# Attention on transposed 64x64 tiles, its root spread by DMA, in a fused attention and two-expert kernel

## The chip, the cores and the metric

One Trainium2 chip, one core of it. The metric is the device time of one launch in microseconds, the median of three runs.

## What is computed

Linear attention over 8 batches, 8 heads, 576 rows, 64 columns a head, an RMS norm over each head's 64 columns, a gated layer with a product over the rows, then a convolution layer, all in fp32.

```python
kv = einsum('bhsd,bhse->bhde', k, v)
o = einsum('bhsd,bhde->bhse', q, kv)
x = o / sqrt(mean(o * o, -1) + 1e-6) * g_norm          # heads joined: (8, 576, 512)
h = relu(x @ w_in); u, v = halves of h
v_n = (v - mean(v)) / sqrt(var(v) + 1e-6)
x = (u * (w_spatial @ v_n + b_spatial)) @ w_out        # first layer
h = relu(x @ w_in2)
c = convolution of h over the rows, 3 taps
out = (h * sigmoid(c)) @ w_out2                        # second layer
```

## The kernel before, in words

The program is written by hand, one instruction list for each engine, tied by semaphores: what stands in a list runs in that order, and a wait holds everything behind it on its engine. `PE` is TensorE, `DVE` VectorE, `ACT` ScalarE, `POOL` GpSimd, and `SP` the queue that issues the loads and stores.

The products of the two layers are made of three products each (`PASSES`): both factors are split into a high part (a copy rounded to fp32r, `HI`) and a low part (the rest, `LO`). The attention's own products are plain fp32. Each plain fp32 matmul leaves two MATMUL and two LDWEIGHTS records in the trace, a transpose or an fp32r matmul one of each.

The program has three stages. **The prologue** (to 44.4 us) loads and splits the weights, multiplies `w_out` by `w_in2` (`W`, L435 and `w_product`, 96 matmuls of 512 columns) and begins the attention of batch 0. **The first stage** (to about 457 us) is `body(b)` for the eight batches: the value product `v_product(b, i)` in five tiles of rows (L358), the product `u_product(b, m)` in four tiles of columns and the product over the rows `spatial_product(b, m)` in four (both L337), with the attention of batch b+1 laid between them. **The second stage**, to the end, is the second layer; it has no attention.

In the attention of a batch, `kv_product` makes k^T v for a pair of heads at a time on the whole 128x128 array (L312, 20 matmuls of 128 columns); `kv_copy` (L796) takes the two diagonal blocks out. `o_product(a, i)` multiplies 128 rows of q by it (L323, 4 matmuls; five times a batch), rows on the partitions. ACT copies and squares the result (L541, L543), DVE sums each head's squares (L802), forms the mean, takes the root's inverse with one Newton step (L812 to L820), ACT has made the root (L548), and DVE scales the rows (L823). `x_transpose(a, i)` (L330, 4 a time) turns them, since the layer's product wants columns on the partitions; ACT makes the high part (L558) and DVE the low part (L833) with the factor g. In `body` of TensorE, `attend(b + 1)` hands out one of these pieces ahead of `u_product(b, 2)` and one ahead of each `spatial_product`, the last transpose in the next body. SP loads k and v of batch b+2 and q once the products that read them are done, and stores each gated tile (`store_gated`, into a scratch in DRAM).

A bank group written by one product waits for its readers: `spatial_product(b, 3)` for `gate(b, 0)`, the value product for `gate` of the batch before.

## Time and profile before

| | |
|---|---|
| median of three runs | 862.21 us (861.88 to 862.80) |
| the profiled execution, its own time | 862.53 us |
| its span, first to last instruction | 860.3 us |
| TensorE busy | 840.8 us, 98% |
| VectorE, ScalarE, GpSimd busy | 501.5, 394.3, 42.1 us |
| chain that ended last | TensorE 96% |
| granted TensorE clock, mean | 0.994 |

Busy time of TensorE is modelled: each record is longer than the distance to the next one's start, since matmuls overlap in the pipeline. What a matmul costs a full TensorE is read from the starts. The time between the span and the execution's own time, 2.2 us, is launch and end.

### The profile page before, as it was taken

How to read it: one execution, taken by the hardware profiler on the slowest of the kernel's cores; microseconds unless marked ns; L12 is line 12 of the kernel's file. 1: busy time of each engine (PE TensorE's matmuls, PEld its weight loads, DVE VectorE, ACT ScalarE, POOL GpSimd, SP SyncE). 2: the span in 40 equal slices, each digit the busy share in tenths (PEclk: the TensorE clock that was granted, in tenths of full speed). 3: DMA queues.
4: the chain of work that ended last, by engine and by line, in shares of the span. 5: the costliest groups of instructions: out<-in, count | busy, mean ns of one | idle time of the engine just before them, and what ended most of it. 6: DMA issues, size and time to landing. Idle time of an engine off the chain costs nothing.

```text
span 860.3 us, 14580 instructions
## 1 busy us (share of the span) xinstructions
PE 840.8 (98%) x5408; PEld 781.4 (91%) x5408; DVE 501.5 (58%) x1184; ACT 394.3 (46%) x718; POOL 42.1 (5%) x42
## 2 busy tenths in 40 slices
PE   6969999999999999999999999999999999999998
PEld 5859989899998999999899899898989989898996
DVE  3577775756767576675746828174561828347380
ACT  5435343342434434344354637274552738356461
POOL 4151000000000000000022000000000000000000
PEclk9979999999999999999999999999999999999999
DMA  9812322233302323221202030120203020120101
GB/s 312 276 56 85 97 76 93 93 110 110 109 28 82 123 96 110 81 84 70 83 26 86 1 105 2 54 63 37 69 13 104 0 100 4 40 76 3 46 0 61
DMA packets 26276, 65.88 MB, mean 77 GB/s; under 512 B 2050, under 2 KB 2050, under 8 KB 24196
## 3 DMA queue, kind: packets, MB, share of 16 engines
q1 hardware_dynamic: 26100, 65.45, 22.2%
q8 instruction: 19, 0.31, 0.1%
q14 instruction: 13, 0.11, 0.0%
q10 hardware_dynamic: 144, 0.01, 0.0%
HBM read 46.58 MB, written 18.87 MB: 76 GB/s over the span
## 4 chain that ended last, share of the span: by engine, by line
PE 96%; DVE 1%; POOL 1%; ACT 1%; DMA 0%; issue 0%; SPq 0%; POOLq 0%; ACTq 0%; DVEq 0%
PE ps L337 49%; PE ps L492 23%; PE ps L358 11%; PE ps L312 4%; PE ps L323 4%; PE ps L330 2%; PE ps L435 2%; PE ps L447 1%; POOL w_in_split L285 1%; DMA sq_xn<-w_in_dram 0%; POOL w_in_split L276 0%; POOL w_in_split L280 0%; DVE sq_xn L823 0%; DVE ssq L802 0%; DVE rm L816 0%
## 5 line engine op out<-in xcount | busy, mean ns | idle before, releaser
L337 PEld LDWEIGHTS ps<-x_gated_split,w_product_split 128*128 128x128 f32 x1536 | 204.3, 188 | 0.5
L337 PE MATMUL ps<-x_gated_split,w_product_split 128*128 128x288 f32 x1536 | 204.8, 295 | 0.0
L492 PE MATMUL ps<-w_in_split,v_hg_split 128*128 128x512 f32 x832 | 194.6, 390 | 0.0
L492 PEld LDWEIGHTS ps<-w_in_split,v_hg_split 128*128 128x128 f32 x832 | 155.8, 188 | 31.9
L961 DVE SCALAR_TENSOR_TENSOR work<-work,const_cols 128x576 f32<-128x576 f32 x64 | 52.4, 819 | 150.0 <-ACT work L733 149.9
L337 PE MATMUL ps<-w_sp_split,v_hg_split 128*128 128x288 f32 x896 | 126.0, 298 | 0.0
L337 PEld LDWEIGHTS ps<-w_sp_split,v_hg_split 128*128 128x128 f32 x896 | 120.0, 188 | 0.0
L337 PE MATMUL ps<-x_gated_split,w_in_split 128*128 128x288 f32 x768 | 105.5, 297 | 0.0
L337 PEld LDWEIGHTS ps<-x_gated_split,w_in_split 128*128 128x128 f32 x768 | 102.5, 188 | 0.2
L358 PE MATMUL ps<-w_in_split,x_gated_split 128*128 128x512 f32 x384 | 94.3, 402 | 2.0 <-POOL w_in_split L276 2.0
L358 PEld LDWEIGHTS ps<-w_in_split,x_gated_split 128*128 128x128 f32 x384 | 73.1, 194 | 17.2 <-POOL w_in_split L276 2.2
L728 ACT ACTIVATE work<-ps 128x576 f32<-128x576 f32 x64 | 41.8, 653 | 70.6 <-PE ps L337 57.2
L802 DVE TENSOR_REDUCE ssq<-sq_xn 128x8 f32<-128x512 f32 (+1 forms) x40 | 27.4, 684 | 74.8 <-ACT sq_xn L543 74.7
L764 ACT ACTIVATE sq_xn<-ps 128x512 f32<-128x512 f32 x32 | 19.1, 598 | 85.0 <-PE ps L492 85.0
L541 ACT ACTIVATE sq_xn<-ps 128x512 f32<-128x512 f32 (+1 forms) x40 | 23.8, 595 | 64.2 <-PE ps L323 64.2
L967 DVE SCALAR_TENSOR_TENSOR work<-work,const_cols 128x576 f32<-128x576 f32 x64 | 52.1, 815 | 0.6
L733 ACT ACTIVATE work<-work,const_cols 128x576 f32<-128x576 f32 x64 | 49.9, 779 | 2.1
L972 DVE TENSOR_TENSOR work<-work 128x576 f32<-128x576 f32 x64 | 48.2, 753 | 0.1
L567 ACT ACTIVATE work<-ps 128x512 f32<-128x512 f32 x32 | 19.1, 598 | 57.8 <-PE ps L358 46.5
L843 DVE BATCH_NORM_STATS2 bn_stats<-work 128x6 f32<-128x512 f32 (+1 forms) x40 | 27.6, 689 | 28.1 <-ACT work L567 22.5
L978 DVE TENSOR_TENSOR v_hg_split<-work,v_hg_split 128x512 fp32r<-128x512 f32 x64 | 43.9, 685 | 0.0
L738 ACT ACTIVATE work<-work 128x576 f32<-128x576 f32 x64 | 42.9, 670 | 0.0
(90 smaller groups left out, 847.3 us busy)
## 6 DMA issues: line engine op xcount, KB each, us to landing
kv_raw<-kv_main_dram SPq DMA_DIRECT2D x8, 2048.0 KB, 8.7
q_raw<-q_T_dram SPq DMA_DIRECT2D x8, 1152.0 KB, 5.9
gated_scratch<-work SPq DMA_DIRECT2D x32, 288.0 KB, 2.1
q_raw<-gated_scratch SPq DMA_DIRECT2D x8, 1152.0 KB, 5.5
out_dram<-sq_xn SPq DMA_DIRECT2D x32, 256.0 KB, 2.0
work<-w_in_dram SPq DMA_DIRECT2D x3, 1024.0 KB, 8.2
kv_raw<-kv_rest_dram SPq DMA_DIRECT2D x8, 256.0 KB, 9.0
kv_raw<-w_out_dram SPq DMA_DIRECT2D x1, 2048.0 KB, 8.1
```

Source lines behind the costliest of these rows:

```text
L312: last = pe.matmul(PS[:, OB, n], KV[:, 0, j, n], KV[:, 1, j, n], start=(j == 0), stop=(j == NT - 1))
L323: last = pe.matmul(PS[:, OB, m * P:(m + 1) * P], QP[:, o:o + P], kvbd[:, m, :], start=True, stop=True)
L337: last = pe.matmul(pair[bank][:, c, :], st, mo[:, c * HALF:(c + 1) * HALF], start=(n == 0), stop=(n == len(steps) - 1))
L358: last = pe.matmul(dst, x, w, start=(n == 0), stop=(n == len(st) - 1))
L492: last = pe.matmul(PS[:, ROW_BANK[i], :], x, wout2[:, w, f, :], start=(f == 0 and n == 0), stop=(f == FT - 1 and n == len(PASSES) - 1))
L728: act.activation(whole(h_sb[f % 3][:, 1:S + 1]), pair[f % 3], ACT.Relu).then_inc(s_hr, 1)
L733: act.activation(t_sb[f % 2], h_sb[f % 3][:, 1:S + 1], ACT.Copy, scale=cols[:, FT + f:FT + f + 1]).then_inc(s_t0, 1)
L738: act.activation(p_sb[f % 2], t_sb[f % 2], ACT.Sigmoid).then_inc(s_sig, 1)
L961: dve.scalar_tensor_tensor(out=t, in0=h[:, 0:S], scalar=cols[:, f:f + 1], in1=t, op0=ALU.mult, op1=ALU.add).then_inc(s_cv1, 1)
L967: dve.scalar_tensor_tensor(out=t, in0=h[:, 2:S + 2], scalar=cols[:, 2 * FT + f:2 * FT + f + 1], in1=t, op0=ALU.mult, op1=ALU.add).then_inc ...
L972: dve.tensor_tensor(p_sb[f % 2], h_sb[f % 3][:, 1:S + 1], p_sb[f % 2], ALU.mult).then_inc(s_mul, 1)
L978: dve.tensor_tensor(hg[LO][:, f, :], p_sb[f % 2][:, 0:w], hg[HI][:, f, :].bitcast(F32), ALU.subtract).then_inc(s_hlo, 1)
```

## The change

All of the attention is rewritten so that it gives o transposed, with the head's columns on the partitions:

- `kv_product` makes one head at a time, 64x64, the two heads of a pair in the left and right half of the array's columns (40 matmuls of 64 columns a batch, same bank, other partitions). ACT and DVE copy the blocks, each twice (to partitions 0 to 63 and 64 to 127).
- `o_product(a, m)` makes o^T for a pair of heads: four matmuls of 64x64 weights and 288 columns, for two halves of the rows (on the array's two halves of rows) and two heads (on its two halves of columns). 16 a batch. They write banks 6 and 7, which ACT copies to `o_T` (`o_copy`) before the next m.
- ACT squares `o_T` (`square`). `square_sum(a, m)` sums the squares over the partitions by a matmul with a matrix of ones in one column (`sel`): eight matmuls of 64 rows by 32 columns of weights and 144 moving columns, each in another eighth of the array, 32 a batch, into banks 4 and 5.
- There are no transposes. The inverse root is made once a batch on 128x288 elements, written to a scratch in DRAM by four DMAs, and read back by two DMAs that give each of the 64 partitions of a head the same row (`spread_r`). DVE then scales `o_T` by it and by g (`x_scale`, four of 576 elements); ACT makes the high part (`x_hi`), POOL the low part (`x_lo`) and the left-over rows (`x_rows_left`).
- On TensorE `kv_product(b + 1)` stands at the body's start, and `o_product` and `square_sum` between the value products. Their waits are put on the last matmul of the value product ahead of them. Body 0 has an order of its own (`first_body`); the batches 1 to 6 are the loop, batch 7 has no attention to make.
- On SP k, v and q of batch 0 are loaded ahead of the last halves of the weights, and the root of batch 0 is waited for between weight loads.
- Eleven plain fp32 matmuls on zeros start as soon as DVE has filled them, before the weights are there (`s_warm`).
- The buffers of the old path are gone or laid over others; banks change (`V_BANK`).

The core of the diff:

```diff
+V_BANK = [0, 1, 2, 3, 2]
 ROW_BANK = [6, 7, 4, 6, 7]
+KV_BANK, SSQ_BANK, O_BANK = 5, 4, 6
...
+        sq = sb("o_squared", [P, 2, S])
+        rB = sb("r_spread", [P, MT, S])
+        sel = sb("head_select", [P, MT, 32])
+        ms, std, r0 = (sb(n, [P, CH, QS]) for n in ("ms", "std", "r0"))
...
+            def spread_r(a):
+                sp.wait_ge(s_r, a + 1)
+                for g in range(4):
+                    sp.dma_start(r_dram[a, :, :, g * QS:(g + 1) * QS].rearrange("c m t -> m c t"),
+                                 r0[g * 32:g * 32 + MT, :, :]).then_inc(s_rst, DMA)
+                sp.wait_ge(s_rst, (a + 1) * 4 * DMA)
+                for c in range(CH):
+                    rows = r_dram[a, c].rearrange("m s -> (m s)").partition_broadcast(D)
+                    sp.dma_start(rB[c * D:(c + 1) * D, :, :].rearrange("p m s -> p (m s)"), rows).then_inc(s_rB, DMA)
...
+            load_w0(0)
+            load_w0(1)
             load_kv(0)
             load_q(0)
+            load_w0(2)
+            load_w0(3)
+            sp.dma_start(w2_raw[1], w2[:, :, F1:F2]).then_inc(s_w21_in, DMA)
+            sp.wait_ge(s_woT, MT)
+            sp.dma_start(wv_raw, w[:, :, F1:F2]).then_inc(s_win_in, DMA)
+            spread_r(0)
...
             with sp.Fori(0, B - 2) as b:
                 sp.wait_ge(s_kv, b + 2)
                 load_kv(b + 2)
-                store_gated(b, 0, 2)
-                sp.wait_ge(s_o, (b + 2) * NT)
+                sp.wait_ge(s_o, (b + 2) * MT)
                 load_q(b + 2)
-                store_gated(b, 2, MT)
+                spread_r(b + 1)
+                store_gated(b, 0, MT)
...
+            def x_lo(a, m):
+                pool.wait_ge(s_xhi, a * MT + m + 1)
+                pool.tensor_tensor(XG[:, LO, m, :], o_T[:, m, :], XG[:, HI, m, :].bitcast(F32), ALU.subtract).then_inc(s_x, 1)
+
+            def x_rows_left(a):
+                pool.wait_ge(s_xhi, (a + 1) * MT)
+                left = slice(FULL * P, S)
+                pool.tensor_tensor(x_rest[:, :, REST:P], o_T[:, :, left], XG[:, HI, :, left].bitcast(F32), ALU.subtract)
+                pool.tensor_copy(x_rest[:, :, 0:REST], XG[:, HI, :, left].bitcast(F32)).then_inc(s_xr, 1)
...
+            with pool.Fori(2, B) as a:
+                for m in range(MT):
+                    x_lo(a, m)
+                x_rows_left(a)
...
             def kv_product(a):
-
                 pe.wait_ge(s_kv_in, (a + 1) * KV_LOADS * DMA)
-                pe.wait_ge(s_sq, a * NT)
-                for hp in range(MT):
-                    n = slice(hp * P, (hp + 1) * P)
+                for m in range(MT):
                     for j in range(NT):
-                        last = pe.matmul(PS[:, OB, n], KV[:, 0, j, n], KV[:, 1, j, n], start=(j == 0), stop=(j == NT - 1))
+                        for c in range(CH):
+                            n = slice((m * CH + c) * D, (m * CH + c + 1) * D)
+                            last = pe.matmul(PS[c * D:(c + 1) * D, KV_BANK, m * D:(m + 1) * D], KV[:, 0, j, n], KV[:, 1, j, n],
+                                             start=(j == 0), stop=(j == NT - 1))
                 last.then_inc(s_kv, 1)
 
-            def o_product(a, i):
-                if i == 0:
+            def o_ready(a, m):
+                if m == 0:
                     pe.wait_ge(s_q_in, (a + 1) * DMA)
-                    pe.wait_ge(s_kvbd, a + 1)
-                else:
-                    pe.wait_ge(s_sq, a * NT + i)
-                for m in range(MT):
-                    o = m * S + i * P
-                    last = pe.matmul(PS[:, OB, m * P:(m + 1) * P], QP[:, o:o + P], kvbd[:, m, :], start=True, stop=True)
+                    pe.wait_ge(s_kvd0, a + 1)
+                    pe.wait_ge(s_kvd1, a + 1)
+                pe.wait_ge(s_oc, a * MT + m)
+
+            def o_product(a, m):
+                if isinstance(a, int):
+                    o_ready(a, m)
+                for half in (0, 1):
+                    r = slice(half * D, (half + 1) * D)
+                    for c in range(CH):
+                        last = pe.matmul(PS[c * D:(c + 1) * D, O_BANK + half, 0:HALF], kvd[r, m, c, :], QR[r, m, c, :],
+                                         start=True, stop=True)
                 last.then_inc(s_o, 1)
 
-            def x_transpose(a, i):
-                pe.wait_ge(s_norm, a * NT + i + 1)
-                pe.wait_ge(s_x, a * NT + i)
-                for m in range(MT):
-                    last = pe.transpose(PS[:, TB, m * P:(m + 1) * P], xn[i % 2][:, m * P:(m + 1) * P], ident[:, :])
-                last.then_inc(s_xtp, 1)
+            def square_ready(a, m):
+                pe.wait_ge(s_sq, a * MT + m + 1)
+
+            def square_sum(a, m):
+                if isinstance(a, int):
+                    square_ready(a, m)
+                for g in range(4):
+                    for c in range(CH):
+                        r = slice(c * D, (c + 1) * D)
+                        last = pe.matmul(PS[g * 32:(g + 1) * 32, SSQ_BANK + c, 0:QS], sel[r, m, :], sq[r, m % 2, g * QS:(g + 1) * QS],
+                                         start=(m == 0), stop=(m == MT - 1))
+                last.then_inc(s_ssq, 1)
...
                 for n, (x, w) in enumerate(st):
+                    if n == len(st) - 1 and ahead and not isinstance(b, int):
+                        if i < MT:
+                            o_ready(b + 1, i)
+                        if i:
+                            square_ready(b + 1, i - 1)
...
             def body(b, ahead):
-                first = isinstance(b, int) and b == 0
+                if ahead:
+                    pe.wait_ge(s_g, b * MT - 2)
+                    kv_product(b + 1)
                 for i in range(NT):
-                    if i == 2:
-                        x_transpose(b, 4)
-                    v_product(b, i)
-                    if first and i == 0:
-                        o_product(0, 4)
-                        x_transpose(0, 3)
-                if ahead and not first:
-                    kv_product(b + 1)
-                if first:
-                    pe.wait_ge(s_winu, MT)
-                u_product(b, 0)
-                u_product(b, 1)
-                pieces = attend(b + 1) if ahead else iter(())
-                if first:
-                    kv_product(1)
-                    u_product(b, 2)
-                    next(pieces)
-                else:
-                    next(pieces, None)
-                    u_product(b, 2)
-                u_product(b, 3)
-                if first:
-                    pe.wait_ge(s_sp_lo, NT)
-                    pe.wait_ge(s_b, 1)
+                    v_product(b, i, ahead)
+                    if ahead:
+                        if i < MT:
+                            o_product(b + 1, i)
+                        if i:
+                            square_sum(b + 1, i - 1)
                 for m in range(MT):
-                    next(pieces, None)
+                    u_product(b, m, ahead)
+                for m in range(MT):
                     spatial_product(b, m)
...
+            pe.wait_ge(s_warm, 1)
+            for n in range(11):
+                pe.matmul(PS[:, O_BANK, 0:P], sq[:, 0, 0:P], sq[:, 0, 0:P], start=True, stop=True)
+            for j in (0, 1):
...
+            def o_copy(a, m):
+                act.wait_ge(s_o, a * MT + m + 1)
+                if not (isinstance(a, int) and a == 0):
+                    act.wait_ge(s_x, a * MT)
+                    act.wait_ge(s_xr, a)
+                act.activation(whole(o_T[:, m, :]), PS[:, O_BANK:O_BANK + 2, 0:HALF], ACT.Copy).then_inc(s_oc, 1)
+
+            def square(a, m):
+                act.wait_ge(s_oc, a * MT + m + 1)
+                act.wait_ge(s_ssq, a * MT + max(m - 1, 0))
+                act.activation(sq[:, m % 2, :], o_T[:, m, :], ACT.Square).then_inc(s_sq, 1)
+
+            def x_hi(a, m):
+                act.wait_ge(s_xm, a * MT + m + 1)
+                if m == 0:
                     act.wait_ge(s_u, a * MT)
-                src = PS[:, TB, :].rearrange("p (m t) -> p m t", m=MT)[:, :, 0:n]
-                if i == FULL:
-                    act.activation(x_rest[:, :, 0:n], src, ACT.Copy, scale=g_col)
-                act.activation(XG[:, HI, :, i * P:i * P + n], src, ACT.Copy, scale=g_col).then_inc(s_xhi, 1)
+                act.activation(XG[:, HI, m, :], o_T[:, m, :], ACT.Copy).then_inc(s_xhi, 1)
...
+            def square(a, m):
+                dve.wait_ge(s_oc, a * MT + m + 1)
+                dve.wait_ge(s_ssq, a * MT + max(m - 1, 0))
+                dve.tensor_tensor(sq[:, m % 2, :], o_T[:, m, :], o_T[:, m, :], ALU.mult).then_inc(s_sq, 1)
+
+            def mean_square(a):
+                dve.wait_ge(s_ssq, (a + 1) * MT)
+                dve.tensor_scalar(ms[:, :, :], PS[:, SSQ_BANK:SSQ_BANK + CH, 0:QS], 1.0 / D, EPS,
+                                  ALU.mult, ALU.add).then_inc(s_ms, 1)
+
+            def inverse_root(a):
+
+                dve.wait_ge(s_std, a + 1)
+                dve.wait_ge(s_rst, a * 4 * DMA)
+                dve.reciprocal(r0[:, :, :], std[:, :, :]).then_inc(s_nr, 1)
...
+                dve.wait_ge(s_nr, a * 4 + 4)
+                dve.tensor_tensor(r0[:, :, :], r0[:, :, :], std[:, :, :], ALU.mult).then_inc(s_r, 1)
+
+            def x_scale(a, m):
+                if m == 0:
+                    dve.wait_ge(s_rB, (a + 1) * CH * DMA)
+                    dve.wait_ge(s_sq, (a + 1) * MT)
+                dve.scalar_tensor_tensor(out=o_T[:, m, :], in0=o_T[:, m, :], scalar=g_col, in1=rB[:, m, :],
+                                         op0=ALU.mult, op1=ALU.mult).then_inc(s_xm, 1)
...
             def body(b, ahead):
+                if ahead:
+                    kv_copy(b + 1)
                 for i in range(NT):
                     v_stats(b, i)
-                    if isinstance(b, int) and b == 0 and i == 0:
-                        mean_square(0, 4)
-                        x_lo(0, 3)
-                        normalise(0, 4)
                     if i:
                         v_lo(b, i - 1)
-                    if i == 1:
-                        x_lo(b, 4)
                     v_normalise(b, i)
+                if ahead:
+                    mean_square(b + 1)
                 v_lo(b, NT - 1)
-                if isinstance(b, int) and b == 0:
-                    dve.wait_ge(s_b_hi, 1)
-                    dve.tensor_tensor(wspB[96:97, :], b_raw[96:97, :], wspB[96:97, :].bitcast(F32),
-                                      ALU.subtract).then_inc(s_b, 1)
                 if ahead:
-                    kv_copy(b + 1)
-                pieces = attend(b + 1) if ahead else iter(())
-                next(pieces, None)
+                    inverse_root(b + 1)
+                    for m in range(MT):
+                        x_scale(b + 1, m)
                 for m in range(MT):
-                    next(pieces, None)
                     if not ahead and m == 2:
                         gated_lo(0, 0)
                         gated_lo(0, 1)
                     gate(b, m)
```

TensorE, one body of the loop (batches 1 to 6). Before:

```order
L358 MATMUL ps<-w_in_split,x_gated_split 128x512 x12
...
L358 MATMUL ps<-w_in_split,x_gated_split 128x512 x12
...
L330 MATMUL ps<-ident,sq_xn 128x128 x4
...
L358 MATMUL ps<-w_in_split,x_gated_split 128x512 x24
L358 MATMUL ps<-w_in_split,rest_split 128x512 x8
...
L312 MATMUL ps<-kv_raw 128x128 x20
L337 MATMUL ps<-x_gated_split,w_in_split 128x288 x48
...
L323 MATMUL ps<-kv_blocks,q_raw 128x128 x4
L337 MATMUL ps<-x_gated_split,w_in_split 128x288 x24
...
L337 MATMUL ps<-x_gated_split,w_in_split 128x288 x24
...
L323 MATMUL ps<-kv_blocks,q_raw 128x128 x4
L330 MATMUL ps<-ident,sq_xn 128x128 x4
```

Now (L355 is the k^T v product, L372 o^T, L385 the sums of squares, L422 the value product, L393 `u_product` and the product over the rows):

```order
L355 MATMUL ps<-kv_raw 64x64 x40
...
L422 MATMUL ps<-w_in_split,x_gated_split 128x512 x11
...
L422 MATMUL ps<-w_in_split,x_gated_split 128x512
L372 MATMUL ps<-q_raw,kv_double 64x288 x4
L422 MATMUL ps<-w_in_split,x_gated_split 128x512 x11
...
L422 MATMUL ps<-w_in_split,x_gated_split 128x512
L372 MATMUL ps<-q_raw,kv_double 64x288 x4
L385 MATMUL ps<-o_squared,head_select 32x144 x8
L422 MATMUL ps<-w_in_split,x_gated_split 128x512 x11
```

The 20 + 20 + 20 instructions of the attention (two of every three plain fp32) have become 40 + 16 + 32, all plain fp32, in fifteen changes between tiles of the whole array and of parts of it a body, where there was one size.

VectorE, the end of one body of the loop, from the left-over rows' value statistics on. Now:

```order
L890 TENSOR_SCALAR ms<-ps 128x288
L952 TENSOR_TENSOR v_hg_split<-work,v_hg_split 64x512
...
L897 RECIPROCAL r<-std 128x288
...
L899 TENSOR_TENSOR std<-r 128x288
...
L901 TENSOR_TENSOR std<-std,ms 128x288
...
L903 TENSOR_SCALAR std<-std 128x288
...
L905 TENSOR_TENSOR r<-r,std 128x288
...
L911 SCALAR_TENSOR_TENSOR o_x<-o_x,const_cols,r_spread 128x576 x4
...
L957 TENSOR_TENSOR work<-ps,work 128x576
...
L957 TENSOR_TENSOR work<-ps,work 128x576
```

The four scalings by the spread root (L911) stand ahead of the four gates (L957) that the product over the rows and the stores wait for. Before, a gate followed each tile's normalisation (L823), and no DMA was waited for.

The queue of SP, one turn of its loop. Now:

```order
L181 DMA q_raw<-q_T_dram 128x2304
...
L186 DMA r_scratch<-r 4x2x144
...
L186 DMA r_scratch<-r 4x2x144
...
L186 DMA r_scratch<-r 4x2x144
...
L186 DMA r_scratch<-r 4x2x144
...
L191 DMA r_spread<-r_scratch 64x2304
...
L191 DMA r_spread<-r_scratch 64x2304
...
L196 DMA gated_scratch<-work 128x576
```

The root's four writes and two reads stand between the load of q and the stores of the gated tiles.

## Rows read from the trace of the kernel before

**Rows 1.** The page: busy time by engine, and the chain that ended last.

```profile
PE 840.8 (98%) x5408; PEld 781.4 (91%) x5408; DVE 501.5 (58%) x1184; ACT 394.3 (46%) x718; POOL 42.1 (5%) x42
...
PE 96%; DVE 1%; POOL 1%; ACT 1%; DMA 0%; issue 0%; SPq 0%; POOLq 0%; ACTq 0%; DVEq 0%
```

**Rows 2.** Windows, bodies 1 to 6: length, TensorE busy, clock, DMA.

```profile
106.94:158.41 51.47, 51.47 (x367) 1.00 0.27 92
...
364.30:415.77 51.47, 51.47 (x366) 1.00 0.22 80
```

**Rows 3.** Order of time, TensorE, body 1: start us, us, line, count.

```profile
120.15 4.62 PE L312 MATMUL ps<-kv_raw 128*128 128x128 f32 x40
124.53 6.60 PE L337 MATMUL ps<-x_gated_split,w_in_split 128*128 128x288 f32 x48
130.97 1.05 PE L323 MATMUL ps<-kv_blocks,q_raw 128*128 128x128 f32 x8
131.78 6.61 PE L337 MATMUL ps<-x_gated_split,w_in_split 128*128 128x288 f32 x48
138.22 1.05 PE L323 MATMUL ps<-kv_blocks,q_raw 128*128 128x128 f32 x8
139.11 0.60 PE L330 MATMUL ps<-ident,sq_xn 128*128 128x128 f32 x4
139.47 3.96 PE L337 MATMUL ps<-w_sp_split,v_hg_split 128*128 128x288 f32 x28
...
158.41 0.86 PE L358 MATMUL ps<-w_in_split,x_gated_split 128*128 128x512 f32 x3
```

**Rows 4.** Groups by line, TensorE's weight loads: busy us, mean ns.

```profile
L312 PEld LDWEIGHTS ps<-kv_raw 128*128 128x128 f32 x320 | 36.8, 192 | 1.7 <-issue 1.2
L330 PEld LDWEIGHTS ps<-ident,sq_xn 128*128 128x128 f32 x160 | 19.1, 143 | 8.7 <-DVE sq_xn L823 7.7
```

**Rows 5.** Windows, prologue and body 0, TensorE.

```profile
0.00:44.44 44.44, 34.74 (x180) 1.00 0.84 285
44.44:106.94 62.50, 56.79 (x377) 0.92 0.23 78
```

**Rows 6.** Waits of TensorE in the whole span: us, times, longest.

```profile
PE ps L330 <- DVE sq_xn L823: 6.7, 3, 5.7
PE ps L435 <- DVE w_product_split L926: 5.8, 1, 5.8
PE ps L358 <- POOL w_in_split L276: 2.0, 1, 2.0
```

**Rows 7.** Windows: length, TensorE busy, granted clock, DMA share, GB/s.

```profile
5.00:10.00 5.00, 4.17 (x10) 1.00 0.98 324
...
58.00:60.00 2.00, 1.20 (x5) 0.50 0.00 0
...
62.00:64.00 2.00, 2.00 (x10) 0.89 0.00 0
```

**Rows 8.** Groups, first weight product, 5 to 12 us, then 12 to 19.

```profile
L435 PE MATMUL ps<-w_product_split,v_hg_split 128*128 128x512 f32 x16 | 6.4, 583 | 5.8 <-DVE w_product_split L926 5.8
...
L435 PE MATMUL ps<-w_product_split,v_hg_split 128*128 128x512 f32 x33 | 7.7, 390 | 0.0
```

**Rows 9.** Page, DMA issues: count, KB each, median us to landing.

```profile
q_raw<-q_T_dram SPq DMA_DIRECT2D x8, 1152.0 KB, 5.9
gated_scratch<-work SPq DMA_DIRECT2D x32, 288.0 KB, 2.1
```

**Rows 10.** Groups by line, VectorE and GpSimd: busy us, mean ns.

```profile
L961 DVE SCALAR_TENSOR_TENSOR work<-work,const_cols 128x576 f32<-128x576 f32 x64 | 52.4, 819 | 150.0 <-ACT work L733 149.9
L876 DVE TENSOR_TENSOR work<-ps,work 128x576 f32<-128x576 f32 x32 | 24.2, 755 | 12.4 <-PE ps L337 12.3
...
L290 POOL TENSOR_TENSOR w_sp_split<-w_sp_raw,w_sp_split 128x576 fp32r<-128x576 f32 x4 | 5.7, 1419 | 13.8 <-ACT w_sp_split L666 13.8
```

**Rows 11.** Loads of q, issue to landing.

```profile
DMA to landing us min/median/max: 5.2/5.9/16.3
```

458 lines of the change are left out of this document (239 added, 219 removed).

## The prediction

> **What bounds the kernel now.** I read the page first: TensorE is busy 98% of the span and 96% of the chain that ended last, all others at 58% or less [rows 1]. Then the stretches of the first stage: each of bodies 1 to 6 lasts 51.47 us, TensorE is busy in all of it, its clock is granted in full, and the DMA engines are at a quarter [rows 2]. So in the loop only what TensorE executes counts. Then the order of time of one body, for the price of the attention by starts: k^T v 124.53 - 120.15 = 4.38 us for 40 records; the pieces of o, of which a body has five, 0.81 once and then 0.89 each, 4.37 us for 40; the five transposes 0.36 each, 1.8 us for 20 [rows 3]. Together 10.5 us of a body, seven times, and the rest, 41.0 us, is untouched by the change. Last the start, where TensorE does idle: the prologue has 34.7 us of work in 44.4, body 0 lasts 62.5 us, 11.0 more than its sisters, with 56.8 busy [rows 5]. The waits there are 5.8 us for the first weights, 5.7 of the 6.7 before transposes in one wait for VectorE's scaled rows, and 2.0 for GpSimd [rows 6]. Around them the clock is at its lower level: granted 0.50 from 58 to 60 us, 0.89 from 62 to 64 [rows 7]. The second stage is not touched.
>
> **The unit price.** A record of a plain fp32 matmul with 128 columns costs 4.38 / 40 = 0.110 us [rows 3], 0.86 ns a column, and every such matmul leaves two. By columns, then, a record of the new k^T v (64 columns) is 0.055 us, of o^T (288) 0.246, of the sums of squares (144) 0.123. A batch has 80, 32 and 64 of them: 4.4, 7.9 and 7.9 us if they run one after the other. Side by side in the halves, quarters and eighths of the array, they are 2.2, 2.0 and 1.0 us. The trace of before has only tiles of the whole array and shows neither. The bounds of the sum are thus 5.2 and 20.2 us a batch, against 10.5.
>
> **Which value I take.** I take the tiles to run side by side, with three allowances. For k^T v a record is preceded by its weight load, 192 ns for 128 columns, which today just hides under the neighbours at one per 0.110 us [rows 3, 4]; halved it is as long as the halved record, so it may or may not be shared: 3.3 us, the middle of 2.2 and 4.4. For o^T 2.2 us (2.0 and a little for four ends). For the sums of squares a start every 0.015 us would be needed to reach 1.0; the closest starts in the trace are those of the transposes, 0.36 / 4 = 0.09 us [rows 3], which at 64 records would be 5.8 us. I take 2.2, nearer the lower end, since starts at 0.09 are only an upper bound of what issue needs. Then there are fifteen changes of tile size a body. None is in the trace. The lower bound is 0; the upper, from the weight load that can't hide and is followed by its matmul, 0.19 us each [rows 4], 2.9 us in all. I take 0.1 each, 1.5 us. Sum: 3.3 + 2.2 + 2.2 + 1.5 = 9.2 us, 1.3 less than 10.5.
>
> The Trainium skill (TensorEngine Tiling, Key Properties) says that changing the tiling mode drains the array, but gives no time; no run here shows it yet. By it the fifteen changes can't be free.
>
> **The loop.** Six bodies by -1.3: -7.9 us. This holds if nothing new makes TensorE wait. Each cover by name. The copies of k^T v (two of 256 elements on each of two engines, less than the 0.76 us of one with 576 [rows 10]) lie under the first value product, 2.7 us (24 of 512 columns in 5.5). `o_copy` and `square` on ScalarE, priced by the same row at 0.76 us each at most, lie under the next value product, whose last matmul carries the wait; behind that wait stands the whole of TensorE, the margin is about 1 us. The root: the sums end about 21.9 us into the body; mean, root, Newton step and the low part between them are eight instructions of some 0.48 us (288 elements, under two thirds of 0.76 [rows 10]), 3.8 us; the writes 2.1 us and the spread of 1152 KB 5.9 us [rows 9] end it at about 34.5; four scalings of 0.82 [rows 10] end at 37.8. The first gate behind them on VectorE is due when its spatial product is done, at 38.6, and TensorE needs it at 46.2. The low parts, 4 x 1.42 us on GpSimd [rows 10], and the left-over rows end at about 45, and the next value product starts after 53. If that cover of 8 us were gone, the rest would fall on each of seven bodies. On SP the spread stands ahead of the stores, which ScalarE waits for only a body later: nothing. Whatever VectorE and ScalarE are relieved of is worth nothing beside a full TensorE.
>
> **The start.** The first weight product now finds its clock up. Its first 16 records last 583 ns, the later 33 last 390 [rows 8]; 48 matmuls take 13.7 us for 10.9 at the later pace of 0.228. The eleven matmuls on zeros are 22 records at twice 0.110 us, 4.8 us, and end at about 5.7, where the first weights are there. Nothing is behind them. The order of loads: 1.05 MB of weights and 2.36 of k and v at 324 to 428 GB/s [rows 7] are there at about 12.5 us. The prologue's sum: 5.8 of waiting, 96 weight products x 0.228 = 21.9, attention 9.2, a wait of 1.5 for k and v, 4 for copies that nothing covers (`kv_copy`, three times `o_copy` with one pair of banks), ends at 42.4 us. But x of batch 0 needs the seventh piece of W, done 2.7 earlier, then two copies 1.5, four scalings 3.3, the parts 2.1, so the first value product is at 46.6, after an idle of 4 us that lowers the clock again: the window at half clock before cost some 1.7 us each time [rows 7], and I take that. With 1.8 us for waits that I don't see, body 0 begins at 48.4 and takes 41.0 + 9.2 + 1.7, and body 1 begins at 100 instead of 106.9: -6.9. What goes is the stall of 5.7 us for VectorE; what is late next is x.
>
> **Sum.** 862.5 - 7.9 - 6.9 = 847.7 us against the profiled execution (862.53; its span is 860.3, with 2.2 us around it). The median of the runs is 0.3 lower: 847.5, I say 848. Own range of this case 830 to 858.
>
> **Rivals.**
>
> *Two records, one tile: only neighbours overlap.* Each matmul is two records for the same tile, and the second can't start before the first has streamed. If starts keep their order, the next tile's first record can lie only beside this tile's second: each matmul costs one record instead of two, and one at the end. Then o^T is 4 x 5 x 0.246 = 4.9 us, the sums 4 x 9 x 0.123 = 4.4, with 3.3 and 1.5 together 14.1 us a batch, 3.6 more than now. Six bodies: +21.6; the start, with about 1.7 batches of attention 4.9 dearer, -6.9 + 8.3 = +1.4. Time: 885 us, slower. With free changes of tile and k^T v at 2.3 it is 866, so the case decides from two tiles on that can't share. For it: starts are in order in every row of rows 3, and a record's pair is always adjacent. Against it: nothing in the trace but that a part of the array is idle. The Trainium skill (TensorE: Matmul & The Clock Gate, Part 3) states that matmuls keep program order in start and end, and measures side-by-side tiles at 3.07 times for four; it does not say what two passes of fp32 do. By that order the sum would be this rival's.
>
> *No overlap at all.* 20.2 + 1.5 = 21.7 us a batch: six bodies +67, the start -6.9 + 21, so 944 us. For it: only that no row shows tiles side by side.
>
> *The spread is late.* One load of q took 16.3 us to land instead of 5.9 [rows 11]; the spread reads one short row for 64 partitions. At 16.3 us the scalings end at 48.2, the gate that TensorE needs at 46.2 comes at 49, and each of seven bodies stands 3 us: 848 + 21 = 869. Below 13 us it costs nothing.
>
> *The change only moves work*, 10.5 us a batch as before: -6.9 by the start alone, 856.
>
> **How the numbers follow.** Side by side: 0.52. Only neighbours: 0.30. None: 0.08. Late spread: 0.05. Only the start: 0.05. The time is that of the first, 848. The range goes down to 828, a little under its own range (side by side with free changes and cheap k^T v is 5.2 us a batch, 817, and leaves 0.06 out), and up to 890, which holds the neighbours' 885 and leaves out its upper part and the no-overlap case (0.14). A measurement of this kernel tells 0.2% (1.7 us) from no change. Faster by that: 0.52 and 0.04 of the last case; within: 0.04; slower: 0.40.
>
> **What would show it.** Right: in a body of the loop k^T v takes 2.2 to 4.4 us by starts, one o^T with its sums under 1.3, bodies of about 50.2 us without a wait of TensorE, body 1 at about 100 us. The neighbours' rival shows as 1.2 us and 1.1 for them and bodies of 55. The gap from the last matmul of one size to the first of the next, beyond its record's price, is the price of a change. Wrong would be any wait of TensorE in the loop on the sums, the copies, the gate or x; idle of GpSimd or ScalarE is no sign.

## The result: 894.02 us, slower by 3.7%

The changed kernel takes 894.02 us (median of 4 runs, 893.05 to 894.39), the kernel before beside it 862.44 (4 runs, 861.88 to 862.8): ratio 1.0365, 95% interval 1.0347 to 1.0383. The profiled execution of the change has a span of 892.6 us, 32.3 more than before. Forecast were 848 us and a range of 828 to 890: the sign is wrong, and the time lies outside the range.

The page of the change, busy time by engine and the chain that ended last:

```profile
PE 841.5 (94%) x6038; PEld 743.9 (83%) x6038; DVE 456.3 (51%) x903; ACT 383.9 (43%) x666; POOL 100.5 (11%) x89
...
PE 70%; DVE 12%; DMA 7%; issue 5%; ACT 4%; SPq 1%; DVEq 0%; ACTq 0%
```

Against [rows 1], TensorE is busy for the same time, but idle for 51 us instead of 20, and its share of the chain fell from 96 to 70%. VectorE and the DMA engines stand in the chain now. TensorE's waits in the whole span say where:

```profile
PE ps L393 <- DVE work L957: 21.3, 7, 4.0
PE ps L422 <- issue: 6.1, 1, 6.1
PE ps L385 <- ACT o_squared L629: 4.3, 1, 4.3
PE ps L355 <- DMA kv_raw<-kv_rest_dram: 2.9, 1, 2.9
PE ps L508 <- DVE w_product_split L1017: 2.8, 1, 2.8
```

Before, the longest line was 6.7 us and all of it lay in the start [rows 6]. The first line here is a wait of the loop, for `gate` (L957): once in body 0 (0.55 us) and six times in bodies 1 to 6, 3.5 us on average. The windows of body 0, 1 and 3, then of the 10 us before, around and behind one such wait (length, busy time of TensorE, its weight loads, VectorE, ScalarE and GpSimd, granted clock, DMA share, GB/s):

```profile
61.49:121.19 59.70, 53.15 (x441) 45.13 (x441) 31.00 (x68) 23.66 (x43) 21.76 (x19) 0.90 0.43 139
121.19:176.44 55.25, 51.26 (x441) 44.41 (x440) 27.06 (x67) 19.08 (x36) 8.02 (x8) 0.94 0.35 110
231.15:285.78 54.63, 51.18 (x442) 44.32 (x441) 27.07 (x67) 19.09 (x36) 7.59 (x6) 0.94 0.34 108
```

```profile
210.00:220.00 10.00, 10.00 (x77) 10.00 (x76) 0.23 (x1) 0.65 (x1) 0.00 (x0) 1.00 0.54 120
220.00:230.00 10.00, 6.47 (x31) 6.23 (x30) 5.91 (x7) 2.73 (x4) 7.58 (x6) 0.68 0.23 88
230.00:240.00 10.00, 10.00 (x120) 7.96 (x118) 3.71 (x12) 2.78 (x6) 0.00 (x0) 0.98 0.56 192
```

A body is 54.4 us on average (326.55 us for the six) instead of 51.47 [rows 2], and body 1 begins at 121.19 instead of 106.94. Bodies 1 to 6 end at 447.74 instead of 415.77. So 14.3 us were lost in the start and 17.7 in the loop; together 32.0 of the 32.3.

**One body on TensorE**, in order of time (start us, us, line, count), from the end of body 2 on:

```profile
219.75 1.36 PE L393 MATMUL ps<-w_sp_split,v_hg_split 128*128 128x288 f32 x9
224.64 6.58 PE L393 MATMUL ps<-w_sp_split,v_hg_split 128*128 128x288 f32 x28 [3.53 <-DVE work L957]
...
231.15 2.55 PE L355 MATMUL ps<-kv_raw 128*64 128x64 f32 x80
233.63 3.01 PE L422 MATMUL ps<-w_in_split,x_gated_split 128*128 128x512 f32 x12
236.57 0.72 PE L372 MATMUL ps<-q_raw,kv_double 64*64 64x288 f32 x8
237.22 3.03 PE L422 MATMUL ps<-w_in_split,x_gated_split 128*128 128x512 f32 x12
...
240.83 0.48 PE L385 MATMUL ps<-o_squared,head_select 64*32 64x144 f32 x16
241.23 3.04 PE L422 MATMUL ps<-w_in_split,x_gated_split 128*128 128x512 f32 x12
```

The small tiles are the part that went well. By starts k^T v is 2.48 us (before 4.38 [rows 3]), a piece of o^T 0.65, the sums of one 0.40: 2.48 + 4 x 1.05 = 6.7 us a body. The last spatial product is the part that went badly. It waits 3.53 us for VectorE's gate, and then its 28 records take 6.6 us, where the same 28 at the full clock took under 4 [rows 3]. The window of 10 us around it has a mean granted clock of 0.68; from 224.64 to 230 us, behind the wait, it is 0.50, the lower of the two levels.

**Why the gate is late**, VectorE, ScalarE and SyncE's queue in body 2, whose sums end at 196.97:

```profile
202.54 0.44 DVE L890 TENSOR_SCALAR ms<-ps 128x288 f32<-128x288 f32 x1
203.01 0.45 ACT L633 ACTIVATE std<-ms 128x288 f32<-128x288 f32 x1 [2.02 <-DVE ms L890]
204.53 0.69 DVE L952 TENSOR_TENSOR v_hg_split<-work,v_hg_split 64x512 fp32r<-64x512 f32 x1 [1.55 <-ACT v_hg_split L669]
205.25 1.95 DVE L897 RECIPROCAL r<-std 128x288 f32<-128x288 f32 x1
208.57 0.46 DVE L905 TENSOR_TENSOR r<-r,std 128x288 f32<-128x288 f32 x1
209.20 1.61 SPq L186 DMA_DIRECT2D r_scratch<-r  x4
211.83 1.23 SPq L191 DMA_DIRECT2D r_spread<-r_scratch  x2
219.76 4.15 DVE L911 SCALAR_TENSOR_TENSOR o_x<-o_x,const_cols,r_spread 128x576 f32<-128x576 f32 x4 [10.74 <-DMA r_spread<-r_scratch]
223.84 2.07 DVE L957 TENSOR_TENSOR work<-ps,work 128x576 f32<-128x576 f32 x3
```

VectorE makes the mean 5.6 us after the sums, since it stands behind the fifth row group's normalisation. Then it waits 1.55 us for ScalarE's high part, ahead of the low part. The reciprocal takes 1.95 us. The root goes out at 209.2 and the reads of the spread are issued at 211.8. VectorE stands idle for 10.74 us, from the end of the root to the landing of the reads, with four gates queued behind the scalings. The first is needed when the spatial products reach the fourth, at 219.75 + 1.36 = 221.1 us; it ends at 224.6.

### The profile page after: what moved, and what is told of

Its sections match the earlier page's. It is cut to its first block, busy times and chain, and to the rows that moved or that the text cites. A ratio compares the mean times of both kernels' runs of the same rounds, so it can differ in the third digit from the quotient of the medians.

```text
span 892.6 us, 15537 instructions
## 1 busy us (share of the span) xinstructions
PE 841.5 (94%) x6038; PEld 743.9 (83%) x6038; DVE 456.3 (51%) x903; ACT 383.9 (43%) x666; POOL 100.5 (11%) x89
## 4 chain that ended last, share of the span: by engine, by line
PE 70%; DVE 12%; DMA 7%; issue 5%; ACT 4%; SPq 1%; DVEq 0%; ACTq 0%
PE ps L393 32%; PE ps L566 22%; PE ps L422 9%; DMA r_spread<-r_scratch 5%; PE ps L355 2%; DVE o_x L911 2%; PE ps L372 2%; DVE r L897 2%; DMA kv_raw<-kv_rest_dram 1%; PE ps L508 1%; DMA r_scratch<-r 1%; DVE bn_stats L924 1%; ACT o_x L624 1%; PE ps L385 1%; DVE v_hg_split L950 1%
## 5 line engine op out<-in xcount | busy, mean ns | idle before, releaser
L393 PE MATMUL ps<-x_gated_split,w_product_split 128*128 128x288 f32 x1536 | 204.8, 294 | 0.0
L393 PEld LDWEIGHTS ps<-x_gated_split,w_product_split 128*128 128x128 f32 x1536 | 204.3, 188 | 0.5
L393 PE MATMUL ps<-w_sp_split,v_hg_split 128*128 128x288 f32 x896 | 136.3, 317 | 21.3 <-DVE work L957 21.3
L393 PEld LDWEIGHTS ps<-w_sp_split,v_hg_split 128*128 128x128 f32 x896 | 133.8, 209 | 22.9 <-DVE work L957 22.9
L393 PE MATMUL ps<-x_gated_split,w_in_split 128*128 128x288 f32 x768 | 106.1, 298 | 1.1 <-DVE ms L890 0.6
L393 PEld LDWEIGHTS ps<-x_gated_split,w_in_split 128*128 128x128 f32 x768 | 103.7, 190 | 3.8 <-issue 1.8
L422 PE MATMUL ps<-w_in_split,x_gated_split 128*128 128x512 f32 x384 | 97.8, 406 | 6.1 <-issue 6.1
L422 PEld LDWEIGHTS ps<-w_in_split,x_gated_split 128*128 128x128 f32 x384 | 71.7, 192 | 27.2 <-issue 12.3
L292 POOL TENSOR_TENSOR x_gated_split<-o_x,x_gated_split 128x576 fp32r<-128x576 f32 x30 | 49.7, 1685 | 312.5 <-ACT x_gated_split L639 312.5
L810 ACT ACTIVATE work<-ps 128x576 f32<-128x576 f32 x64 | 41.8, 654 | 71.1 <-PE ps L393 59.7
L911 DVE SCALAR_TENSOR_TENSOR o_x<-o_x,const_cols,r_spread 128x576 f32<-128x576 f32 x32 | 33.2, 1101 | 74.6 <-DMA r_spread<-r_scratch 74.6
L846 ACT ACTIVATE o_x<-ps 128x512 f32<-128x512 f32 x32 | 19.1, 598 | 85.0 <-PE ps L566 85.0
L639 ACT ACTIVATE x_gated_split<-o_x 128x576 fp32r<-128x576 f32 x32 | 21.9, 684 | 78.3 <-DVE o_x L911 77.5
L957 DVE TENSOR_TENSOR work<-ps,work 128x576 f32<-128x576 f32 x32 | 22.8, 747 | 47.5 <-PE ps L393 47.5
```

Source lines behind the costliest of these rows:

```text
L292: pool.tensor_tensor(XG[:, LO, m, :], o_T[:, m, :], XG[:, HI, m, :].bitcast(F32), ALU.subtract).then_inc(s_x, 1)
L393: last = pe.matmul(pair[bank][:, c, :], st, mo[:, c * HALF:(c + 1) * HALF], start=(n == 0), stop=(n == len(steps) - 1))
L422: last = pe.matmul(dst, x, w, start=(n == 0), stop=(n == len(st) - 1))
L810: act.activation(whole(h_sb[f % 3][:, 1:S + 1]), pair[f % 3], ACT.Relu).then_inc(s_hr, 1)
L911: dve.scalar_tensor_tensor(out=o_T[:, m, :], in0=o_T[:, m, :], scalar=g_col, in1=rB[:, m, :], op0=ALU.mult, op1=ALU.mult).then_inc(s_xm, 1)
```

## The experiments

**1. The gates in front.** `gate(b, 0)` and `gate(b, 1)` need nothing of the spread. The same edit is made in body 0.

```diff
+                gate(b, 0)
+                gate(b, 1)
                 if ahead:
                     for m in range(MT):
                         x_scale(b + 1, m)
-                for m in range(MT):
+                for m in (2, 3):
```

> VectorE's gates 0 and 1 stand ahead of the four scalings, nothing else changes. Theory (queue): TensorE waits 3.4 us a body for gate 0 only because it is queued behind scalings that wait for the spread, and loses 2.7 more in the last spatial product to the lower clock. Both go, a body falls from 54.6 to 48.5 us, perhaps 49.0 where the x parts on GpSimd come out last, and the whole by 6 x 6.1 = 37 us, to 857. Rival (spread itself): the x of the next batch comes no earlier, so TensorE's wait only moves to the next value product: body 53 or more, 885. Rival (tiles): bodies are long by what the tiles cost TensorE: no change, 894.

Measured: 867.11 us (10 runs, 861.74 to 870.23), ratio 1.0048 (1.0028 to 1.0068). The gate's wait is gone from TensorE's list, and two moved gates give back 27 of the 32 us. The loop came out nearly as expected: bodies 1 to 6 take 49.1 us on average, against 48.5 to 49.0. Another wait took part of the old one's place, of value products for the low parts of x:

```profile
PE ps L422 <- POOL x_gated_split L292: 6.7, 6, 2.6
```

Five of the six are in the loop, 0.62 to 1.16 us each: with the gates in front, scalings and low parts end that much later. The sixth, 2.59 us, is ahead of body 7's first value product, and behind it, from 418.7 to 425 us, the granted clock is 0.73. From body 7 on this profile takes 449.2 us, that of the change 444.9. That is some 4 of the 10 us above the expected 857.

**2. The root in front of the last low part as well.**

```diff
                     mean_square(b + 1)
-                v_lo(b, NT - 1)
-                if ahead:
                     inverse_root(b + 1)
+                v_lo(b, NT - 1)
```

> As the run with the gates first, and VectorE's root step (five instructions on 288 elements) also ahead of the last low part of v, so that the root leaves some 2 us earlier. Queue theory: if x was last by half a microsecond in the former run, it no longer is: body 48.5, 854 to 857. Spread rival: 2 us a body less than the former run, 873. Tiles rival: 894.

Measured: 859.06 us (10 runs, 855.83 to 861.94), ratio 0.9967 (0.9951 to 0.9982). Faster than before, by 0.3%, and 2 us or more above the expectation. The loop of this kernel, from one body's k^T v to that of the next:

```profile
310.75 2.55 PE L355 MATMUL ps<-kv_raw 128*64 128x64 f32 x80
...
359.05 1.15 PE L355 MATMUL ps<-kv_raw 128*64 128x64 f32 x32
```

48.30 us, without a wait: 3.2 less than the kernel before. So the attention costs 10.5 - 3.2 = 7.3 us of TensorE, 6.7 in rows and 0.6 left for the changes of tile size. The one wait for the low parts that is left, 1.6 us, is in body 7.

This pair also shows how far the start moves from one execution to another. Experiments 1 and 2 have the same instructions up to the end of body 0. The first value product of body 0, in the profile of experiment 1 and then of 2:

```profile
62.67 8.16 PE L422 MATMUL ps<-w_in_split,x_gated_split 128*128 128x512 f32 x24 [6.18 <-issue]
```

```profile
58.62 8.07 PE L422 MATMUL ps<-w_in_split,x_gated_split 128*128 128x512 f32 x24 [6.21 <-issue]
```

They are 4 us apart with nothing changed ahead of them, and the granted clock from 10 to 30 us is 0.83 in the one and 0.99 in the other. The profile of experiment 2 is the fastest of its ten runs. So what an edit of the start is worth can't be read from two profiles by where body 1 begins; the medians, or the length of body 0 alone, must be compared.

**3. No spread.** The six DMAs of the root's way through memory are left out, and the scalings take o itself as the factor, so x isn't the reference's. The order is the change's, gates behind the scalings.

> The six DMAs of the spread are left out and the scalings use o itself as the factor, so x is not the reference's; order on all engines as in the change. Queue theory and spread rival both: the scalings run as soon as the root is made, gate 0 is ready with its product, body 48.5, 857 or a little less if the start gains too. If DMA traffic of the spread slows other things, lower still. Tiles rival: 894. Together with the gates-first run it tells whether the order alone hides the 10.7 us that the scalings wait.

Measured: 856.3 us (4 runs, 854.66 to 859.1), ratio 0.9942 (0.9922 to 0.9962), bodies of 48.3 us (214.85 to 263.17) with no wait in the loop. Without the spread the order does no harm; with it, the order does. But body 1 begins at 118.20, only 3.0 us earlier than in the change, less than the start moves by itself: most of the 14.3 us of the start isn't the spread, and TensorE still waits 5.87 us ahead of the first value product.

**4. Without the warm-up.** Eleven matmuls less.

> The eleven matmuls on zeros are left out. Theory: the first 24 weight products take 8 us or more instead of 5.7, but TensorE waits 2.9 us for k and v behind them, so the time moves by under 1 us. Rival (warm-up matters): 3 us later, 897, or more, since the clock has to be raised again.

Measured: 893.08 us (4 runs, 892.74 to 894.87), ratio 1.0364 (1.0346 to 1.0381), so the warm-up is worth nothing here. The first 24 records of the weight product in the change, then without warm-up:

```profile
5.84 5.73 PE L496 MATMUL ps<-w_product_split,v_hg_split 128*128 128x512 f32 x24
14.47 3.78 PE L355 MATMUL ps<-kv_raw 128*64 128x64 f32 x80 [2.90 <-DMA kv_raw<-kv_rest_dram]
```

```profile
5.74 7.22 PE L496 MATMUL ps<-w_product_split,v_hg_split 128*128 128x512 f32 x24 [5.74 <-DVE w_product_split L1008]
14.82 2.55 PE L355 MATMUL ps<-kv_raw 128*64 128x64 f32 x80 [1.86 <-DMA kv_raw<-kv_rest_dram]
```

The weight product does gain 1.5 us, and gives them to the wait for k and v, which land at about 14.5 to 14.8 in both. In the profile with the warm-up k^T v also runs at the slower clock (0.62 granted from 14.5 to 18.2 us, against 1.00), and takes 3.78 us instead of 2.55. That isn't a fixed price of the warm-up: experiment 2 has it too, and its k^T v takes 2.55 us behind 2.78 of waiting.

**5. Another order at the start.** As 2, and batch 0's o^T and sums stand in one piece behind its k^T v, ahead of the second half of the weight product, their copies, squares and root likewise on ScalarE and VectorE.

```diff
             o_product(0, 1)
+            square_sum(0, 0)
             o_product(0, 2)
-            w_product0(2, 0)
-            w_product0(2, 1)
+            square_sum(0, 1)
             o_product(0, 3)
-            w_product0(2, 2)
-            square_sum(0, 0)
-            w_product0(2, 3)
-            square_sum(0, 1)
             square_sum(0, 2)
...
```

> On the version with gates and root first, the whole attention of batch 0 stands on TensorE directly behind its k^T v, ahead of the second half of the first weight product, and copies, squares and root follow on ScalarE and VectorE; the scalings of batch 0 stand behind six pieces of W, not seven. Theory (x of batch 0 is late at the start because its root is made late and is spread for 10 us): the root leaves at about 32 us instead of 40, TensorE's wait of 6.2 us ahead of the first value product is under 2, and some 2 us more are lost between the pieces of o; body 0 starts at 51 to 53 us instead of 58.6, the whole is 851 to 853. Rival (the start is bound by the loads and the slower clock): body 0 starts at 57 or later, 858.

Measured: 850.97 us (4 runs, 848.94 to 851.94), ratio 0.9861 (0.9845 to 0.9877), 8.1 us under the median of experiment 2. The time is the expected one, the theory behind it is not. Body 0 begins at 55.71 us, not at 51 to 53, and TensorE still waits 5.80 us for x, not under 2. What is gone from its list are the waits of 2.8 and 0.7 us for VectorE's and GpSimd's splits. The trace of the change shows that the spread never was what held x of batch 0:

```profile
54.17 4.15 DVE L911 SCALAR_TENSOR_TENSOR o_x<-o_x,const_cols,r_spread 128x576 f32<-128x576 f32 x4 [0.17 <-DMA r_spread<-r_scratch]
```

VectorE waits 0.17 us for it there, since the scalings stand behind the seventh piece of W; they and two low parts (3.15 us) are what TensorE waits for. In experiment 5, where they stand behind six pieces, the wait for the spread is 2.56 us.

**6. As 5, and in body 0** the last copy and square of batch 1 stand on ScalarE ahead of the fifth row group's high part.

```diff
+                o_copy(1, 3)
+                square(1, 3)
                 v_hi(0, NT - 1)
                 b_hi()
                 u_relu(0, 0)
-                o_copy(1, 3)
-                square(1, 3)
```

> As the run with the start's order, and in body 0 ScalarE copies and squares the last piece of o ahead of its wait for VectorE's last v and of the bias. Theory: TensorE's wait of 4.3 us for that square goes, with the lower clock behind it some 5 us: 846 to 849, ahead of the kernel before by 1.6%. Rival: the wait moves to the first spatial product, 851 to 853.

Measured: 848.51 us (5 runs, 848.39 to 854.18), ratio 0.9861 (0.9836 to 0.9887), which can't be told from experiment 5. In the profile the wait of 4.3 us is gone, but 3.2 us for the mean (L883 there) stand in its place: the rival's mechanism, though the time lies in the theory's range. Body 0 is 56.8 us long instead of 58.0.

**7. k^T v with one head's five matmuls in a row** instead of the two heads in turn. On experiment 2:

```diff
                 for m in range(MT):
-                    for j in range(NT):
-                        for c in range(CH):
+                    for c in range(CH):
+                        for j in range(NT):
```

> On the version with gates and root first, k^T v issues the five matmuls of one head in a row, all in the same half of the array's columns, then the other head's. Theory A (matmuls start in program order, so only those next to each other in the list can lie side by side): k^T v takes 4.0 to 4.4 us instead of 2.5, 7 x 1.7 = 12 us more in all, 870. Theory B (each part of the array takes its own from far ahead in the list): 2.5 us still, 859.

Measured: 866.22 us (4 runs, 865.29 to 867.12), ratio 1.0046 (1.0031 to 1.0062). The same 80 records:

```profile
318.75 3.62 PE L355 MATMUL ps<-kv_raw 128*64 128x64 f32 x80
322.31 3.02 PE L422 MATMUL ps<-w_in_split,x_gated_split 128*128 128x512 f32 x12
```

3.56 us by starts instead of 2.48, 1.08 more, and bodies of 49.4 (269.34 to 318.75) instead of 48.3. Seven times 1.08 is 7.6 us, and the medians are 7.2 apart. The product's time lies between the two expectations: the order of the tiles in the program counts for 1.1 us, and some overlap is left beyond that of next neighbours, for which theory A gave 4.0 us or more. What k^T v takes without any overlap was not measured.

**8. The root far earlier, gates left where they are.** In the change's order only mean, root and reciprocal with the four instructions behind it move, ahead of the fifth row group, in the loop, on VectorE and ScalarE.

```diff
                 for i in range(NT):
+                    if ahead and i == NT - 1:
+                        mean_square(b + 1)
+                        inverse_root(b + 1)
                     v_stats(b, i)
```

> The change with one edit: in the loop the mean, the root and the seven instructions behind them stand ahead of the fifth row group's statistics instead of behind them, on VectorE and ScalarE; the gates stay behind the four scalings, the start and body 0 are as in the change. If the gate is late because the root is queued and the spread merely long (theory), the spread is issued some 6.5 us earlier (reads at about 14.9 - 6.5 = 8.5 us after the end of the sums), the scalings end near 35 us into the body, before the 38 to 39 at which the first spatial product is done, TensorE's 3.5 us wait for the gate goes from the six bodies of the loop and stays in body 0, and the time is about 894 - 6 x 6.3 = 856 to 859 us. If the landing of the spread were at fault (it lands when the DMA engines are free, however early it is issued), the wait shrinks by less than half and the time stays over 875. A price may appear: the fifth group's low part now comes about 4 us later, just before TensorE reaches it; if it is late, a wait of up to 1 us a body, +6.

Measured: 896.67 us (4 runs, 895.19 to 897.24), ratio 1.0395 (1.0379 to 1.0411). The expectation missed by 38 us, yet its mechanism is there. Sums end at 197.72:

```profile
197.72 3.44 PE L393 MATMUL ps<-x_gated_split,w_in_split 128*128 128x288 f32 x24
...
204.44 0.63 ACT L656 ACTIVATE work<-work 64x512 f32<-64x512 f32 x1 [3.90 <-DVE work L922]
205.12 12.23 PE L393 MATMUL ps<-x_gated_split,w_in_split 128*128 128x288 f32 x72 [3.96 <-ACT work L656]
206.62 1.23 SPq L191 DMA_DIRECT2D r_spread<-r_scratch  x2
214.85 3.00 DVE L911 SCALAR_TENSOR_TENSOR o_x<-o_x,const_cols,r_spread 128x576 f32<-128x576 f32 x4 [4.86 <-DMA r_spread<-r_scratch]
217.19 15.01 PE L393 MATMUL ps<-w_sp_split,v_hg_split 128*128 128x288 f32 x112
221.17 0.76 DVE L957 TENSOR_TENSOR work<-ps,work 128x576 f32<-128x576 f32 x1 [3.31 <-PE ps L393]
```

The reads are issued 8.9 us after the sums instead of 14.9, the scalings are over before the first spatial product, the 112 records of the four spatial products run without a gap, and VectorE waits for TensorE. The median landing is 6.4 us, as in the change (6.6). But VectorE's addition for the fifth row group (L922), the last reader of its bank, now stands behind the root, ScalarE's step (L656) behind that, and TensorE waits 3.96 us for it: a wait of the same length at another place, 24.4 us in all, 0.5 of them in body 0 as in the change.

**9. The best order, and body 0's mean and root ahead of its last low part** (on experiment 6: `mean_square(1)`, `inverse_root(1)` ahead of `v_lo(0, NT - 1)`, and `root(1)` ahead of `b_hi()`).

> The best order so far (gates and root first, attention at the start in one piece, body 0's last copy and square early) with body 0's mean and root also ahead of its last low part. TensorE's 3.23 us wait for the mean in body 0 should shrink to under 1 us, and the slower clock behind it with it: body 1 begins 3 to 4 us earlier and the time is 844 to 846 us. If something else comes due in its place (the low part of the fifth group or of the bias row, then 5 us later), the time stays at 848 to 850.

Measured: 846.44 us (5 runs, 844.43 to 847.9), ratio 0.9814 (0.9798 to 0.9831). The wait for the mean falls from 3.23 to 0.62 us and nothing stands in its place in body 0, which is 52.8 us long instead of 56.8: the 3 to 4 us expected. Body 1 begins only 1.4 us earlier in this profile, since body 0 itself begins 2.6 us later, behind the same instructions. It is the best kernel of this study, 1.9% faster than the one before.

**10. As 8, with the reciprocal and what follows behind the fifth group's statistics**, only the mean ahead of them.

> As e8_root_early, but only the mean stands ahead of the fifth row group's statistics; the reciprocal and the four instructions behind it follow the statistics. In e8 the wait for the gate was gone from the loop, and TensorE waited 3.96 us a body for ScalarE's last reader of the fifth group's bank instead, because VectorE's reader stood behind the root. Here that reader comes right behind the mean. Theory (the change is slow in the loop only because the gate behind the scalings is 3.5 us late): the spread is issued some 4.3 us earlier than in the change, the last scaling ends at about 219.6 where TensorE wants the gate at 221, no wait of TensorE is left in bodies 1 to 6, their length is 48.3 to 49, and the time is 856 to 860 us. If a wait of up to 1 us a body for the bank is left, 862 to 866. If a fourth wait takes the place and the body stays at 54, so that the order of the gates is the only cure, 894.

Measured: 879.28 us (4 runs, 879.09 to 881.2), ratio 1.0208 (1.0191 to 1.0225), 20 us above the expectation. TensorE's waits:

```profile
PE ps L393 <- ACT work L674: 11.9, 6, 2.0
...
PE ps L393 <- ACT work L656: 5.5, 7, 1.0
```

Again no wait for the gate, and again others, 3 us a body in two pieces: 0.8 to 1.0 us for the bank, and 2.0 us for ScalarE's ReLU of the first tile of u (L674), queued behind the fifth group's high part, which waits for VectorE's normalisation behind the root. Bodies take 51.6 to 53.4 us.

## Why the prediction was wrong

**The unit price: right in mechanism, too high in size.** Forecast was 9.2 us a body for the attention, measured 7.3. k^T v is 2.48 (taken 3.3, lower bound 2.2), o^T 2.6 (2.2), the sums 1.6 (2.2), the changes of size some 0.6 for all fifteen (1.5). The body of experiment 2 is the forecast case, without a wait, and with 48.3 us instead of 50.2 it would have been worth -19 us in the loop, not -7.9. What the Trainium skill (TensorEngine Tiling, Key Properties) says of a drain at each change agrees with the trace in that 12 records of a value product take 2.94 us by starts between small tiles, where 24 took 5.5 in the trace of before: 0.2 us for the two changes at their ends. That it is the drain, and not the wait on the product's last matmul, wasn't tested.

**Rival "only neighbours overlap": refuted as written.** It gave 1.2 us to a piece of o^T, whose four tiles take 0.65. In windows of 0.1 us four records of it start together. Experiment 7 shows what is true of it: the order of the tiles counts. Its time, 885, came near the measured one by luck, for another reason.

**The step that failed in the loop: "gate 0 is due at 38.6, TensorE needs it at 46.2".** The prediction named the right place and the right point for a stall, with a margin of 8 us, and called it safe. By rows, from the start of body 2 at 176.44, the scalings end at 47.4 us into the body instead of 37.8, and TensorE needs the gate at 44.7 instead of 46.2. The 9.6 us are made up so, less 0.8 that the prediction's sum held without a term (21.9 + 3.8 + 2.1 + 5.9 is 33.7, it says 34.5):

- The sums end at 20.5, 1.4 earlier than the 21.9 forecast.
- Mean to the corrected root 12.1 us (196.97 to 209.03), forecast 3.8. Of the 8.3 more, 5.6 are queueing of the mean on VectorE behind the fifth row group, of which the sum held nothing, 1.5 the reciprocal, priced at 0.48 as an addition of its size and measured at 1.95, and most of the rest the 1.55 us for ScalarE's high part.
- Writes and spread 10.7 us to the first scaling (209.03 to 219.76), forecast 2.1 + 5.9. Writes and their wait are 2.6 us, and from the issue of the reads to the scaling it is 7.9, of which one read's landing is 6.6 at the median.
- The scalings 4.15 us, forecast 3.3.

The rival "the spread is late" saw this stall and its 3 us a body, but hung it on a landing time of over 13 us, which didn't come. The landing took 6.6 us where 5.9 were forecast; the rest of the way to the gate made the difference.

**What the wait cost, beyond itself.** The prediction's rival priced a stall at its length. Each wait of 3.5 us also took some 2.7 us of slower clock behind it: 48.3 + 3.5 + 2.7 = 54.5, where 54.4 were measured. The prediction knew that price from the start of the kernel before (1.7 us) and didn't carry it to the loop.

**The step that failed at the start: -6.9 us, measured +14.3.** The prologue's sum counted work at the full clock and 1.8 us for waits that it did not see. Body 0 begins at 61.5 us instead of 48.4, and lasts 59.7 instead of 51.9. The trace shows waits of 2.9 us for k and v (1.5 forecast), 1.2, 0.8 and 0.9 for copies, 0.7 for a square, 1.9, 0.8 and 2.8 for splits, and 6.1 for x (4 forecast, with scalings at 3.3 us that took 4.15 and parts at 2.1 that took 3.15). Behind the longer ones the clock is at its lower level: granted 0.50 from 44.5 to 48 us and from 61.5 to 65. Body 0 has 4.3 us for a square behind two of ScalarE's splits, and 0.50 behind it, from 96 to 100. A shorter product that is waited for as often isn't a shorter start. The warm-up, credited through a first product at the full clock, is worth nothing (experiment 4).

How large the step is holds to some 2 us only: in the five profiles that have the change's instructions up to there (the change and experiments 1, 2, 8 and 10) body 0 begins at 58.6 to 62.7 us. The order of the start and of body 0 does matter beyond that. By the medians experiment 5 wins 8.1 us, 6 can't be told from it, and 9 wins 2.1 more; by the length of body 0, 6 wins 1.2 and 9 wins 3.9.

**What is shown and what is open.** Shown: the loop's loss is the wait for the gate that is queued behind the spread's scalings (experiments 1 and 3), and with that gone the tiles are worth 3.2 us a body (2). Experiments 8 and 10 show that the spread doesn't land late when it is issued early, and that an earlier root is no cure by itself: VectorE and ScalarE have no slack at the fifth row group, though they are busy 51 and 43% of the span, and what is put ahead pushes something else behind TensorE's need. How the start's loss divides between the order of the loads, the waits and the clock was not taken apart; nor was why the clock in the start differs between executions of the same instructions. The last 5.5 us of waiting for x stand in the best kernel too.

## What to carry to other kernels

A margin on a path over three engines and a DMA must be summed with the queue each instruction stands in, not only with its own duration: here 3.8 us of arithmetic took 12.1. When a new long wait enters an in-order queue, first move ahead of it whatever doesn't depend on it and is needed soon; two lines gave back 27 us here. Price a stall of a full TensorE with the slower clock behind it, which nearly doubled it. And before an edit is credited with microseconds, see how far two executions of the same instructions differ at that place: here it was 4 us.

## What was not expected of the hardware

A reciprocal on VectorE of 128x288 takes 1.95 us, where a product of the same shape takes 0.46.

VectorE's short instructions are stretched in the start. The same line L901, in body 2 and then at the start, where GpSimd works at the same time:

```profile
207.73 0.46 DVE L901 TENSOR_TENSOR std<-std,ms 128x288 f32<-128x288 f32 x1
```

```profile
39.61 1.42 DVE L901 TENSOR_TENSOR std<-std,ms 128x288 f32<-128x288 f32 x1
41.06 1.28 DVE L903 TENSOR_SCALAR std<-std 128x288 f32<-128x288 f32 x1
42.38 1.52 DVE L905 TENSOR_TENSOR r<-r,std 128x288 f32<-128x288 f32 x1
```

A cause was not tested. GpSimd's presence alone isn't enough: L899, a product of the same shape, took 0.46 us at 39.12 with GpSimd at work. The three stretched ones end at 41.03, 42.34 and 43.90 us, each 0.2 to 0.3 us behind the end of the subtraction that GpSimd was in when they began (40.71, 42.18, 43.58), as if they had waited for it. GpSimd's own subtraction of 128x576 has a mean of 1.69 us in the change, against 1.42 for one of 128x576 before [rows 10].

Four tiles of a quarter of the array do run together, in two rounds: in windows of 0.1 us over one piece of o^T (first the matmuls in flight, then the weight loads) four matmuls are in flight, and four more come about 0.25 us later, the second record of each pair.

```profile
236.50:236.60 0.10, 0.03 (x4) 0.03 (x4) 1.00 0.44 164
236.60:236.70 0.10, 0.10 (x4) 0.10 (x8) 1.00 0.58 246
236.70:236.80 0.10, 0.10 (x4) 0.08 (x8) 1.00 0.39 164
236.80:236.90 0.10, 0.10 (x8) 0.00 (x0) 1.00 0.39 164
```
